# Two blocks of routing arithmetic moved ahead of the first expert tile: the "gate" and "slot row" steps on the Vector engine, and the writes of their results on the Scalar engine's queue

## The chip, the cores and the metric

The kernel runs on one core of one Trainium2 chip. A core has five engines with a queue of instructions each: the tensor engine (PE; its weight loads are listed as PEld), the Vector engine (DVE), the Scalar engine (ACT), GpSimd (POOL) and the Sync engine (SP), which here only starts transfers. Engines run side by side and wait for one another through semaphores. The metric is the device time of one execution in microseconds (us).

## The reference

Three networks in a row, all in 32-bit floating point, on 8 x 576 = 4608 tokens of width 512 (8 heads of 64):

```python
p_packed = sm_attn(p, k, v)              # 32 packed queries per head look at 576 keys
x = sm_attn(q, p_packed, p_packed)       # 576 queries look at the 32 packed rows
# mixture of experts: 8 experts, each token goes to one
logits = x @ w_gate
expert_idx = np.argmax(logits, axis=1)
probs = softmax(logits); gate_w = probs[token, expert_idx]
for e in range(8):
    out[mask_e] = gate_w[mask_e] * (relu(x[mask_e] @ w1[e]) @ w2[e])    # 512 -> 1024 -> 512
# dense layer
h = out @ w_in                           # 512 -> 2048
return (s * relu(h)**2 + b) @ w_out      # 2048 -> 512
```

## The kernel before

There are three stages, and each is written out for every engine as its own program.

**Attention** (up to about 187 us). 16 units of 4 heads. Along with it the expert of each token is picked, and GpSimd scatters the token rows to a table in DRAM that is sorted by expert (`scatter`, L408).

**Experts** (about 214 to 723 us). The sorted table is cut into slots of 128 rows, 40 of them for these inputs, and each slot belongs to one expert. For a slot `s` the work is a ring:

- Scalar starts the load of the 128 rows (`load(s)`, L854), after reading the row number from a table into a register (L853).
- The tensor engine turns them (`slot_in(s)`, L656).
- Scalar copies the turned rows, rounded to the matmul format, to `xT_hi` (`x_hi(s)`, L858), and Vector subtracts that from the exact values to give `xT_lo` (`x_lo(s)`, L1166). Products of both parts are summed, three matmuls for each product (`split_mm`, L647 to L649).
- The tensor engine multiplies by the first weights (`slot_up(s)`: 24 matmuls in two halves), Scalar applies relu to each half (`relu(s)`, L863), the tensor engine turns the result (`slot_turn`, L691), Scalar and Vector split it (`h_hi`, L868, and `h_lo`, L1172), and the tensor engine multiplies by the second weights (`slot_down`).

`slot_up(s)` waits for `x_lo(s)`, as the semaphore `xlo_done` says. The order on the tensor engine is fixed by the program: slot_in(0), slot_up(0), slot_in(1), slot_turn(0), then a loop of slot_up(s), slot_in(s+1), slot_down(s-1), slot_turn(s).

The weights are split into a high and a low part in the same manner, 8 chunks for an expert. The first ten chunks are split by Scalar (`round_high`, L812) together with GpSimd or, for the last three of them, Vector (`round_low`, L1144). All later ones are GpSimd's (`split`, L389 and L391, two instructions a chunk on SBUF). It may start expert 2 only when expert 0's last slot is through (`release`).

**Routing arithmetic** between the two stages, on Vector. Each instruction is wrapped in `step`, which makes the next instruction wait on the semaphore `rt` until this one has ended. Two groups of it are what the change moves:

- the gates, `reduce_sum` (L1153), add of a small constant (L1154), `reciprocal` (L1155), which need the exponentials that Scalar makes at L888;
- the slot rows, four instructions on a table of 96 x 48 x 7 (L1158, L1160, L1161, L1162), which need only the row number of each token.

Scalar writes both results to DRAM with three transfers each (L899, L902). They are read back at the end of the expert stage only. In this kernel the gates stand on Vector behind `x_lo(0)`, and the slot rows behind `h_lo(0)`; Vector also reads the number of slots into a register (L1175) ahead of `x_lo(0)`. On Scalar, both groups of writes stand behind `h_hi(0)`.

**Dense layer** (from about 727 us): gather of the expert results, then 9 groups of 512 tokens.

Of the kernel before, what the change touches and what calls it, by code (L numbers as in the profile page):

```python
# [9 lines left out]
ALU = mybir.AluOpType  # L10
ACT = mybir.ActivationFunctionType
AX = mybir.AxisListType

P = 128
B, H, S, D = 8, 8, 576, 64
NPK = 32
E = 8
SP_ = 96
# [12 lines left out]
EPS = 1e-9  # L31
# [4 lines left out]
C = N // SP_  # L36
# [18 lines left out]
def build(nc, q, k, v, p, w_gate, w1, w2, w_in, w_out, s_in, b_in, out):  # L55
    rows_dram = nc.dram_tensor("x_by_expert", [E * REG, DM], F32).ap()
    ys_dram = nc.dram_tensor("y_by_slot", [SLOTS * P, DM], F32).ap()
    pos_dram = nc.dram_tensor("slot_row_of_token", [N, 1], I32).ap()
    gate_dram = nc.dram_tensor("gate_of_token", [N, 1], F32).ap()

    ctx = ExitStack()
    with ctx:
        def sb(name, shape, dt=F32, scope=ctx):
            return scope.enter_context(nc.sbuf_tensor(name, shape, dt))

        def sem(name):
            return ctx.enter_context(nc.semaphore(name))
# [30 lines left out]
        eoff = sb("expert_region", [SP_, E])  # L98
# [11 lines left out]
        pos_i = sb("row_of_token_sb", [SP_, C], I32)  # L110
# [36 lines left out]
        c = ExitStack()  # L147
# [7 lines left out]
        mxa = sb("mxa", [SP_, C], scope=c)  # L155
        dl = sb("dl", [SP_, C, E], scope=c)
        el = sb("el", [SP_, C, E], scope=c)
        gate = sb("gate", [SP_, C], scope=c)
# [4 lines left out]
        doff = sb("doff", [SP_, E - 1], scope=c)  # L163
        pos_e = sb("pos_e", [SP_, C, E - 1], scope=c)
        pos_s = sb("pos_s", [SP_, C], scope=c)
        slot_row = sb("slot_row_of_token_sb", [SP_, C], I32, scope=c)
# [8 lines left out]
        c = ExitStack()  # L175
# [55 lines left out]
        rt = sem("rt")  # L231
        rexp = sem("rexp")
        zeros_done, zeroed = sem("zeros_done"), sem("zeroed")
        pos_out, gate_out, tok_in = sem("pos_out"), sem("gate_out"), sem("tok_in")
# [531 lines left out]
        def _(act):  # L766
# [80 lines left out]
            def token_rows(t, c):  # L847
                return t.rearrange("(b p c j) o -> c p b (j o)", b=B, c=3, j=J)[c]


            def load(s):

                row = act.value_load(x_at[0:1, bass.ds(s, 1)], min_val=0, max_val=E * REG - P)  # L853
                act.dma_start(xin[:], rows_dram[bass.ds(row, P), :]).then_inc(xin_in, 16)  # L854

            def x_hi(s):
                act.wait_ge(tx_full, s + 1)
                nc.scalar.copy(xT[0][:], ps[:, TXB, :]).then_inc(xhi_done, 1)  # L858
# [6 lines left out]
            def h_hi(s):  # L865
                for n in range(2):
                    act.wait_ge(th_full, 2 * s + n + 1)
                    nc.scalar.copy(hT[0][:, n * 512:(n + 1) * 512], ps[:, THB + n, :]).then_inc(hhi_done, 1)  # L868
# [19 lines left out]
            nc.scalar.activation(el[:], dl[:], ACT.Exp).then_inc(rexp, 1)  # L888
            x_hi(0)
            load(1)  # L890
            act.wait_ge(tail_zero, 16)

            relu(0)
            x_hi(1)
            load(2)
            h_hi(0)
            act.wait_ge(rt, RT_GATE)
            for c in range(3):
                act.dma_start(token_rows(gate_dram, c), gate[c * NPK:(c + 1) * NPK, :].rearrange("p (b j) -> p b j", b=B)).then_inc(gate_out, 16)  # L899
            act.wait_ge(rt, RT_ROW)  # L900
            for c in range(3):
                act.dma_start(token_rows(pos_dram, c), slot_row[c * NPK:(c + 1) * NPK, :].rearrange("p (b j) -> p b j", b=B)).then_inc(pos_out, 16)  # L902
            with act.Fori(1, before3 + 1) as s:
                relu(s)
                x_hi(s + 1)
# [71 lines left out]
        def _(dve):  # L977
# [122 lines left out]
            def step(ins, mark=None):  # L1100

                done[0] += 1
                ins.then_inc(rt, 1)
                dve.wait_ge(rt, done[0])
                if mark is not None:
                    assert mark == done[0], (mark, done[0])
# [33 lines left out]
            def round_low(n):  # L1140
                dve.wait_ge(hi_done, n + 1)
                dve.wait_ge(conv, n)
                at = n // NCH * WBUF
                nc.vector.tensor_tensor(part(at, 1, n % NCH * CH, CH), raw[n % 2][:], part(at, 0, n % NCH * CH, CH), ALU.subtract).then_inc(conv, 1)  # L1144
# [3 lines left out]
            step(nc.vector.tensor_tensor(dl[:], lg[:], over_e, ALU.subtract), RT_DL)  # L1148
            round_low(EARLY)
            round_low(EARLY + 1)  # L1150
            def gates():
                dve.wait_ge(rexp, 1)
                step(nc.vector.reduce_sum(mxa[:], el[:], AX.X))  # L1153
                step(nc.vector.tensor_scalar_add(mxa[:], mxa[:], EPS))  # L1154
                step(nc.vector.reciprocal(gate[:], mxa[:]), RT_GATE)  # L1155

            def slot_rows():
                step(nc.vector.tensor_tensor(pos_e[:], pos_i[:].unsqueeze(2).to_broadcast([SP_, C, E - 1]),  # L1158
                                             eoff[:, 1:].unsqueeze(1).to_broadcast([SP_, C, E - 1]), ALU.is_ge))
                step(nc.vector.tensor_tensor(pos_e[:], pos_e[:], doff[:].unsqueeze(1).to_broadcast([SP_, C, E - 1]), ALU.mult))  # L1160
                step(nc.vector.reduce_sum(pos_s[:], pos_e[:], AX.X))  # L1161
                step(nc.vector.tensor_tensor(slot_row[:], pos_i[:], pos_s[:], ALU.subtract), RT_ROW)  # L1162

            def x_lo(s):
                dve.wait_ge(xhi_done, s + 1)
                nc.vector.tensor_tensor(xT[1][:], ps[:, TXB, :], xT[0][:], ALU.subtract).then_inc(xlo_done, 1)  # L1166

            def h_lo(s):
                for n in range(2):
                    cols = slice(n * 512, (n + 1) * 512)  # L1170
                    dve.wait_ge(hhi_done, 2 * s + n + 1)
                    nc.vector.tensor_tensor(hT[1][:, cols], ps[:, THB + n, :], hT[0][:, cols], ALU.subtract).then_inc(hlo_done, 1)  # L1172

            dve.wait_ge(tables, 1)
            before3 = dve.value_load(slots_m3[0:1, 0:1], min_val=N // P - 3, max_val=SLOTS - 3)  # L1175
            x_lo(0)
            gates()
            x_lo(1)
            h_lo(0)
            slot_rows()  # L1180
            with dve.Fori(1, before3 + 2) as s:
                x_lo(s + 1)
                h_lo(s)
# [50 lines left out]
RT_GATE = 19  # L1234
RT_ROW = 23
# [21 lines left out]
```

## Time and profile before

| | |
|---|---|
| median of 3 runs | 1572.74 us (1571.44 to 1578.85) |
| the profiled execution's own time | 1572.74 us |
| its span, from first to last instruction | 1571.0 us |
| tensor engine busy | 1471.6 us, 94% of the span |
| Vector busy | 483.4 us, 31% |
| Scalar busy | 468.8 us, 30% |
| GpSimd busy | 408.9 us, 26% |

The span is 1.7 us shorter than the execution's time; what is ahead of the first and behind the last instruction is in the time alone. An engine that isn't the tensor engine costs time only where the tensor engine waits for it, so what is to be looked for is where the tensor engine stands idle and what ended that idle time. Line numbers in rows are those of the kernel before. An instruction's own wait is noted behind it in brackets.

### The profile page before, as it was taken

How to read it: one execution, taken by the hardware profiler on the slowest of the kernel's cores; microseconds unless marked ns; L12 is line 12 of the kernel's file. 1: busy time of each engine (PE TensorE's matmuls, PEld its weight loads, DVE VectorE, ACT ScalarE, POOL GpSimd, SP SyncE). 2: the span in 40 equal slices, each digit the busy share in tenths (PEclk: the TensorE clock that was granted, in tenths of full speed). 3: DMA queues.
4: the chain of work that ended last, by engine and by line, in shares of the span. 5: the costliest groups of instructions: out<-in, count | busy, mean ns of one | idle time of the engine just before them, and what ended most of it. 6: DMA issues, size and time to landing. Idle time of an engine off the chain costs nothing.

```text
span 1571.0 us, 24276 instructions
## 1 busy us (share of the span) xinstructions
PE 1471.6 (94%) x8664; PEld 1180.9 (75%) x8665; DVE 483.4 (31%) x777; ACT 468.8 (30%) x793; POOL 408.9 (26%) x268
## 2 busy tenths in 40 slices
PE   7787549999999999995999999999999999999998
PEld 5565438888888888884788888888888888888886
DVE  4767831111111111111523232232323223232322
ACT  6554212222222222221222232232223222222222
POOL 0343559356275666205600000000000000000000
PEclk9878669999999999997999999999999999999999
DMA  9768465233242343212201000010101001000000
GB/s 276 233 218 237 126 223 166 90 121 117 76 147 94 114 132 107 87 35 94 67 7 41 14 35 13 13 40 7 40 13 40 7 13 40 7 33 0 27 0 27
DMA packets 51917, 124.75 MB, mean 79 GB/s; under 512 B 8224, under 2 KB 14368, under 8 KB 50720
## 3 DMA queue, kind: packets, MB, share of 16 engines
q1 hardware_dynamic: 31904, 83.13, 16.6%
q10 hardware_dynamic: 14016, 22.10, 4.4%
q0 software_dynamic: 5952, 18.88, 3.9%
q8 instruction: 33, 0.54, 0.1%
q14 instruction: 12, 0.10, 0.0%
HBM read 90.76 MB, written 33.33 MB: 79 GB/s over the span
## 4 chain that ended last, share of the span: by engine, by line
PE 92%; DVE 3%; issue 2%; DMA 1%; ACT 1%; POOL 1%; ACTq 0%; DVEq 0%; POOLq 0%; SPq 0%
PE psum L647 18%; PE psum L649 18%; PE psum L648 18%; PE psum L727 9%; PE psum L728 9%; PE psum L729 9%; PE psum L486 2%; PE psum L691 2%; PE psum L715 1%; PE psum L656 1%; PE psum L592 1%; PE psum L550 1%; PE psum L529 1%; PE psum L605 1%; DVE x_rows L1067 1%
## 5 line engine op out<-in xcount | busy, mean ns | idle before, releaser
L1195 DVE SCALAR_TENSOR_TENSOR s_r_r<-r_relu,s_col 128x512 f32<-128x512 f32 x144 | 112.8, 784 | 452.2 <-ACT r_relu L937 452.2
L647 PE MATMUL psum<-weights_split,gT_hi 128*128 128x512 f32 x576 | 229.8, 399 | 1.9 <-DVE gT_lo L1197 1.9
L727 PE MATMUL psum<-yT_hi,weights_split 128*128 128x512 f32 x576 | 228.2, 396 | 1.4 <-issue 1.4
L728 PE MATMUL psum<-yT_lo,weights_split 128*128 128x512 f32 x576 | 228.3, 396 | 0.0
L729 PE MATMUL psum<-yT_hi,weights_split 128*128 128x512 f32 x576 | 228.1, 396 | 0.0
L648 PE MATMUL psum<-weights_split,gT_hi 128*128 128x512 f32 x576 | 227.3, 395 | 0.0
L649 PE MATMUL psum<-weights_split,gT_lo 128*128 128x512 f32 x576 | 227.2, 394 | 0.0
L937 ACT ACTIVATE r_relu<-psum 128x512 f32<-128x512 f32 x144 | 86.0, 597 | 464.4 <-PE psum L729 464.4
L389 POOL TENSOR_TENSOR weights_split<-weights_raw,one 128x1024 fp32r<-128x1024 f32 x70 | 134.7, 1924 | 253.2 <-PE psum L649 236.1
L450 POOL DMA_INDIRECT y_gathered<-y_by_slot,tpos x36 | 34.4, 956 | 579.3 <-PE psum L715 577.3
L391 POOL TENSOR_TENSOR weights_split<-weights_raw,weights_split 128x1024 fp32r<-128x1024 f32 x70 | 169.4, 2419 | 5.5
L1197 DVE SCALAR_TENSOR_TENSOR gT_lo<-s_r_r,b_col,gT_hi 128x512 fp32r<-128x512 f32 x144 | 112.7, 783 | 114.1 <-ACT gT_hi L940 114.1
L940 ACT ACTIVATE gT_hi<-s_r_r,b_col 128x512 fp32r<-128x512 f32 x144 | 104.3, 724 | 123.3 <-DVE s_r_r L1195 123.3
L647 PE MATMUL psum<-weights_split,xT_hi 128*128 x320 | 130.6, 408 | 2.9 <-DVE xT_lo L1166 2.9
L647 PE MATMUL psum<-weights_split,hT_hi 128*128 x320 | 129.5, 405 | 2.5 <-DVE hT_lo L1172 2.5
L727 PEld LDWEIGHTS psum<-yT_hi,weights_split 128*128 128x128 f32 x576 | 108.7, 189 | 27.9 <-issue 1.8
L647 PEld LDWEIGHTS psum<-weights_split,gT_hi 128*128 128x128 f32 x576 | 108.3, 188 | 27.4 <-issue 2.1
L729 PEld LDWEIGHTS psum<-yT_hi,weights_split 128*128 128x128 f32 x576 | 108.7, 189 | 26.2
L728 PEld LDWEIGHTS psum<-yT_lo,weights_split 128*128 128x128 f32 x576 | 108.6, 189 | 26.2
L649 PEld LDWEIGHTS psum<-weights_split,gT_lo 128*128 128x128 f32 x576 | 108.1, 188 | 25.7
L649 PE MATMUL psum<-weights_split,xT_lo 128*128 x320 | 127.3, 398 | 0.0
L648 PE MATMUL psum<-weights_split,xT_hi 128*128 x320 | 127.1, 397 | 0.0
(142 smaller groups left out, 1796.8 us busy)
## 6 DMA issues: line engine op xcount, KB each, us to landing
weights_raw<-in_moe_w_dram SPq DMA_DIRECT2D x64, 512.0 KB, 3.4
x_slot<-x_by_expert ACTq DMA_DIRECT2D x40, 256.0 KB, 2.7
y_by_slot<-y_slot ACTq DMA_DIRECT2D x40, 256.0 KB, 2.0
k_sb<-in_k_dram SPq DMA_DIRECT2D x16, 576.0 KB, 6.7
q_sb<-in_q_dram SPq DMA_DIRECT2D x16, 576.0 KB, 7.2
v_sb<-in_v_dram SPq DMA_DIRECT2D x48, 192.0 KB, 5.6
out_dram<-out_sb SPq DMA_DIRECT2D x9, 1024.0 KB, 3.8
weights_raw<-in_moe_w_in_dram SPq DMA_DIRECT2D x8, 512.0 KB, 3.6
```

Source lines behind the costliest of these rows:

```text
L389: nc.gpsimd.tensor_tensor(hi, raw[c_ % 2][:], one[:].to_broadcast([P, CH]), ALU.mult).then_inc(hi_done, 1)
L391: nc.gpsimd.tensor_tensor(lo, raw[c_ % 2][:], hi, ALU.subtract).then_inc(conv, 1)
L647: nc.tensor.matmul(dst, lhs[0][:, col:col + P], rhs[0], start=first_, stop=False)
L648: nc.tensor.matmul(dst, lhs[0][:, col:col + P], rhs[1], start=False, stop=False)
L649: return nc.tensor.matmul(dst, lhs[1][:, col:col + P], rhs[0], start=False, stop=last_)
L727: nc.tensor.matmul(ps[:, HFB + f % 2, :], w[0], yT[0][:, k_, :], start=(k_ == 0), stop=False)
L728: nc.tensor.matmul(ps[:, HFB + f % 2, :], w[0], yT[1][:, k_, :], start=False, stop=False)
L729: last = nc.tensor.matmul(ps[:, HFB + f % 2, :], w[1], yT[0][:, k_, :], start=False, stop=(k_ == KD - 1))
L937: nc.scalar.activation(rel[:], ps[:, HFB + par, :], ACT.Relu).then_inc(rel_done, 1)
L940: nc.scalar.activation(gT[par][0][:], sq[par][:], ACT.Identity, bias=b_col[:]).then_inc(ghi_done, 1)
L1195: nc.vector.scalar_tensor_tensor(sq[par][:], rel[:], s_col[:], rel[:], ALU.mult, ALU.mult).then_inc(sq_done, 1)
L1197: nc.vector.scalar_tensor_tensor(gT[par][1][:], sq[par][:], b_col[:], gT[par][0][:], ALU.add, ALU.subtract).then_inc(glo_done, 1)
```

## The change

On Vector, the gates and the slot rows lose their functions and stand in the program where these were defined: right behind the last `round_low`, ahead of the register load and of `x_lo(0)`. On Scalar, the six writes with their two waits stand behind `load(1)`, ahead of `relu(0)`. No instruction is added or removed.

```diff
             x_hi(0)
             load(1)
-            act.wait_ge(tail_zero, 16)
-
-            relu(0)
-            x_hi(1)
-            load(2)
-            h_hi(0)
             act.wait_ge(rt, RT_GATE)
             for c in range(3):
                 act.dma_start(token_rows(gate_dram, c), gate[...]).then_inc(gate_out, 16)
             act.wait_ge(rt, RT_ROW)
             for c in range(3):
                 act.dma_start(token_rows(pos_dram, c), slot_row[...]).then_inc(pos_out, 16)
+
+            act.wait_ge(tail_zero, 16)
+
+            relu(0)
+            x_hi(1)
+            load(2)
+            h_hi(0)
             with act.Fori(1, before3 + 1) as s:
...
             round_low(EARLY)
             round_low(EARLY + 1)
-            def gates():
-                dve.wait_ge(rexp, 1)
-                step(nc.vector.reduce_sum(mxa[:], el[:], AX.X))
-                step(nc.vector.tensor_scalar_add(mxa[:], mxa[:], EPS))
-                step(nc.vector.reciprocal(gate[:], mxa[:]), RT_GATE)
-
-            def slot_rows():
-                step(... pos_e, is_ge ...)
-                step(... pos_e, mult ...)
-                step(nc.vector.reduce_sum(pos_s[:], pos_e[:], AX.X))
-                step(... slot_row, subtract ..., RT_ROW)
+            dve.wait_ge(rexp, 1)
+            step(nc.vector.reduce_sum(mxa[:], el[:], AX.X))
+            step(nc.vector.tensor_scalar_add(mxa[:], mxa[:], EPS))
+            step(nc.vector.reciprocal(gate[:], mxa[:]), RT_GATE)
+
+            step(... pos_e, is_ge ...)
+            step(... pos_e, mult ...)
+            step(nc.vector.reduce_sum(pos_s[:], pos_e[:], AX.X))
+            step(... slot_row, subtract ..., RT_ROW)
...
             dve.wait_ge(tables, 1)
             before3 = dve.value_load(slots_m3[0:1, 0:1], ...)
             x_lo(0)
-            gates()
             x_lo(1)
             h_lo(0)
-            slot_rows()
             with dve.Fori(1, before3 + 2) as s:
```

On Vector, the program around the start of the expert stage was this. `mxa` and `el` belong to the gates, `pos_e`, `pos_s` and `slot_row_of_token_sb` to the slot rows, and TENSOR_LOAD is the register load.

```order
L1144 TENSOR_TENSOR weights_split<-weights_raw,weights_split 128x1024 [waits conv,hi_done]
L1175 TENSOR_LOAD slots_minus [waits tables]
L1175 ISA x2
L1166 TENSOR_TENSOR xT_lo<-psum,xT_hi 128x512 [waits xhi_done]
L1153 TENSOR_REDUCE mxa<-el 96x48 [waits rexp]
L1154 TENSOR_SCALAR mxa<-mxa 96x48 [waits rt]
L1155 RECIPROCAL gate<-mxa 96x48 [waits rt]
L1166 TENSOR_TENSOR xT_lo<-psum,xT_hi 128x512 [waits xhi_done,rt]
L1172 TENSOR_TENSOR hT_lo<-psum,hT_hi 128x512 [waits hhi_done] x2
L1158 TENSOR_TENSOR pos_e<-row_of_token_sb,expert_region 96x336
L1160 TENSOR_TENSOR pos_e<-pos_e,doff 96x336 [waits rt]
L1161 TENSOR_REDUCE pos_s<-pos_e 96x48 [waits rt]
```

Now it is this (line numbers are the changed kernel's, one or so off from the ones above). All seven instructions have moved ahead of the first `x_lo`, and the register load between them and it has got the wait for `rt`, the end of the last of the seven, besides the one it had.

```order
L1145 TENSOR_TENSOR weights_split<-weights_raw,weights_split 128x1024 [waits conv,hi_done]
L1153 TENSOR_REDUCE mxa<-el 96x48 [waits rexp]
L1154 TENSOR_SCALAR mxa<-mxa 96x48 [waits rt]
L1155 RECIPROCAL gate<-mxa 96x48 [waits rt]
L1157 TENSOR_TENSOR pos_e<-row_of_token_sb,expert_region 96x336 [waits rt]
L1159 TENSOR_TENSOR pos_e<-pos_e,doff 96x336 [waits rt]
L1160 TENSOR_REDUCE pos_s<-pos_e 96x48 [waits rt]
L1161 TENSOR_TENSOR slot_row_of_token_sb<-row_of_token_sb,pos_s 96x48 [waits rt]
L1175 TENSOR_LOAD slots_minus [waits tables,rt]
L1175 ISA x2
L1166 TENSOR_TENSOR xT_lo<-psum,xT_hi 128x512 [waits xhi_done] x2
```

On Scalar, from the exponential on, before:

```order
L888 ACTIVATE el<-dl 96x384 [waits rt]
L858 CAST xT_hi<-psum 128x512 [waits tx_full]
L854 DMA x_slot<-x_by_expert 128x512
L863 ACTIVATE h_relu<-psum 128x512 [waits h_full,tail_zero]
L863 ACTIVATE h_relu<-psum 128x512 [waits h_full]
L868 CAST hT_hi<-psum 128x512 [waits th_full] x2
L899 DMA gate_of_token<-gate 32x8x6 [waits rt]
L902 DMA slot_row_of_token<-slot_row_of_token_sb 32x8x6 [waits rt]
```

And now:

```order
L888 ACTIVATE el<-dl 96x384 [waits rt]
L858 CAST xT_hi<-psum 128x512 [waits tx_full]
L854 DMA x_slot<-x_by_expert 128x512
L893 DMA gate_of_token<-gate 32x8x6 [waits rt]
L893 DMA gate_of_token<-gate 32x8x6 x2
L896 DMA slot_row_of_token<-slot_row_of_token_sb 32x8x6 [waits rt]
L896 DMA slot_row_of_token<-slot_row_of_token_sb 32x8x6 x2
```

Both groups of writes are now ahead of the first relu, with the two waits for Vector.

## Rows read from the trace of the kernel before

**Rows 1.** Stretches: busy us of PE, PEld, DVE, ACT, POOL; granted clock, DMA share, GB/s.

```profile
199.60:213.90 14.30, 0.00 (x0) 0.00 (x0) 1.22 (x1) 1.67 (x2) 0.92 (x1) 0.50 0.97 318
216.60:221.60 5.00, 4.91 (x12) 3.87 (x13) 1.59 (x3) 0.00 (x0) 4.92 (x3) 0.50 0.54 168
227.40:700.00 472.60, 472.60 (x2266) 387.56 (x2267) 80.05 (x118) 124.98 (x225) 253.07 (x119) 1.00 0.34 108
742.30:747.30 5.00, 4.99 (x12) 3.94 (x13) 0.00 (x0) 0.00 (x0) 4.92 (x3) 0.51 0.20 60
```

**Rows 2.** The chain that ended last, 199 to 225 us: start, duration, what.

```profile
199.70 7.99 DMA x_by_expert<-x_rows,row_of_token_sb
...
215.71 0.70 DVE xT_lo L1166
...
216.69 0.79 PE psum L647
217.48 0.43 PE psum L648
...
222.65 0.23 PE psum L647
```

**Rows 3.** Vector in order of time: start, duration, line, operation.

```profile
214.36 1.22 DVE L1144 TENSOR_TENSOR weights_split<-weights_raw,weights_split 128x1024 fp32r<-128x1024 f32 x1 [2.46 <-ACT weights_split L812]
...
216.32 0.54 DVE L1153 TENSOR_REDUCE mxa<-el 96x48 f32<-96x384 f32 x1
216.89 0.88 DVE L1154 TENSOR_SCALAR mxa<-mxa 96x48 f32<-96x48 f32 x1
217.81 0.45 DVE L1155 RECIPROCAL gate<-mxa 96x48 f32<-96x48 f32 x1
...
228.10 1.08 DVE L1158 TENSOR_TENSOR pos_e<-row_of_token_sb,expert_region 96x336 f32<-96x336 int32 x1
229.21 2.08 DVE L1160 TENSOR_TENSOR pos_e<-pos_e,doff 96x336 f32<-96x336 f32 x1
...
231.86 1.75 DVE L1162 TENSOR_TENSOR slot_row_of_token_sb<-row_of_token_sb,pos_s 96x48 int32<-96x48 int32 x1
```

**Rows 4.** Vector's sequencer, line 1175: durations ns min/median/max, start us.

```profile
L1175 DVEq TENSOR_LOAD <-slots_minus x1: 542/542/542, 214.4 to 214.4; - x1
L1175 DVEq FUSED_REGOPS  x1: 221/221/221, 214.9 to 214.9; - x1
L1175 DVEq SEQ_ASSERT  x1: 35/35/35, 215.2 to 215.2; - x1
```

**Rows 5.** GpSimd in order of time, 215 to 243 us.

```profile
215.84 1.89 POOL L389 TENSOR_TENSOR weights_split<-weights_raw,one 128x1024 fp32r<-128x1024 f32 x1 [15.22 <-DVE weights_split L1144]
217.81 2.37 POOL L391 TENSOR_TENSOR weights_split<-weights_raw,weights_split 128x1024 fp32r<-128x1024 f32 x1
...
226.44 2.38 POOL L391 TENSOR_TENSOR weights_split<-weights_raw,weights_split 128x1024 fp32r<-128x1024 f32 x1
228.77 2.16 POOL L389 TENSOR_TENSOR weights_split<-weights_raw,one 128x1024 fp32r<-128x1024 f32 x1
231.01 2.54 POOL L391 TENSOR_TENSOR weights_split<-weights_raw,weights_split 128x1024 fp32r<-128x1024 f32 x1
...
242.16 1.91 POOL L389 TENSOR_TENSOR weights_split<-weights_raw,one 128x1024 fp32r<-128x1024 f32 x1
```

**Rows 6.** Vector and GpSimd in the attention stage, at 69 us.

```profile
69.30 2.37 POOL L382 TENSOR_TENSOR weights_split<-weights_raw,weights_split 128x1024 fp32r<-128x1024 f32 x1
69.40 2.34 DVE L996 TENSOR_TENSOR eq<-logits,mx 96x48 f32<-96x48 f32 x1
```

**Rows 7.** Scalar and its queue (ACTq) in order of time.

```profile
222.06 0.60 ACT L863 ACTIVATE h_relu<-psum 128x512 f32<-128x512 f32 x1 [6.38 <-PE psum L649]
...
233.64 1.36 ACTq L902 DMA_DIRECT2D slot_row_of_token<-slot_row_of_token_sb  x3
235.19 1.09 ACT L863 ACTIVATE h_relu<-psum 128x512 f32<-128x512 f32 x2 [7.84 <-issue]
```

More of the change, by code:

```diff
@@ L1150, in _ @@
             round_low(EARLY + 1)
-            def gates():
-                dve.wait_ge(rexp, 1)
-                step(nc.vector.reduce_sum(mxa[:], el[:], AX.X))
-                step(nc.vector.tensor_scalar_add(mxa[:], mxa[:], EPS))
-                step(nc.vector.reciprocal(gate[:], mxa[:]), RT_GATE)
-            def slot_rows():
-                step(nc.vector.tensor_tensor(pos_e[:], pos_i[:].unsqueeze(2).to_broadcast([SP_, C, E - 1]),
-                                             eoff[:, 1:].unsqueeze(1).to_broadcast([SP_, C, E - 1]), ALU.is_ge))
-                step(nc.vector.tensor_tensor(pos_e[:], pos_e[:], doff[:].unsqueeze(1).to_broadcast([SP_, C, E - 1]), ALU.mult))
-                step(nc.vector.reduce_sum(pos_s[:], pos_e[:], AX.X))
-                step(nc.vector.tensor_tensor(slot_row[:], pos_i[:], pos_s[:], ALU.subtract), RT_ROW)
+            dve.wait_ge(rexp, 1)
+            step(nc.vector.reduce_sum(mxa[:], el[:], AX.X))
+            step(nc.vector.tensor_scalar_add(mxa[:], mxa[:], EPS))
+            step(nc.vector.reciprocal(gate[:], mxa[:]), RT_GATE)
+            step(nc.vector.tensor_tensor(pos_e[:], pos_i[:].unsqueeze(2).to_broadcast([SP_, C, E - 1]),
+                                         eoff[:, 1:].unsqueeze(1).to_broadcast([SP_, C, E - 1]), ALU.is_ge))
+            step(nc.vector.tensor_tensor(pos_e[:], pos_e[:], doff[:].unsqueeze(1).to_broadcast([SP_, C, E - 1]), ALU.mult))
+            step(nc.vector.reduce_sum(pos_s[:], pos_e[:], AX.X))
+            step(nc.vector.tensor_tensor(slot_row[:], pos_i[:], pos_s[:], ALU.subtract), RT_ROW)
             def x_lo(s):
```

## The prediction

> **What bounds the kernel now.** I read the busy shares first (tensor engine 94%), then the stretches, then the chain, then each engine in order of time around the two places that the change touches. From 227.4 to 700 us the tensor engine is busy for all of 472.6 us, at full granted clock [rows 1]. In that stretch no other engine costs anything, and none can give anything back by being early. The hole is ahead of it: from 199.6 to 213.9 us the tensor engine does nothing, and the granted clock is 0.50, the lower of its two levels [rows 1]. The chain says what ends the hole [rows 2]: GpSimd's last scatter at 199.70 and its transfer of 7.99 us, then the first slot's load, turn and copy, then Vector's x_lo(0) at 215.71 for 0.70, then 0.27 of issue, and at 216.69 the first matmul of slot_up(0). So x_lo(0) is on the path that sets the end. In the kernel before, Vector had nothing in front of it but the last round_low, which starts at 214.36 and takes 1.22 [rows 3]. The seven moved instructions come behind x_lo(0) there, in time in which Vector only waited for others. The change puts them in front of it.
>
> **Where the block starts.** The last round_low ends at 214.36 + 1.22 = 215.58. I start the block at 215.52, as an in-order successor of this instruction overlaps it by some hundredths. The exponentials that it waits for come from Scalar ahead of x_hi(0), so they are there by then.
>
> **How long it takes.** Here the recorded durations can't be copied, as some of them are waiting. L1154 works on 48 elements a partition and is recorded with 0.88; it ends at 216.89 + 0.88 = 217.77 [rows 3]. GpSimd's L389 runs from 215.84 to 217.73 [rows 5]: Vector's instruction ends 0.04 behind it. L1158 ends at 229.18, 0.36 behind the end of GpSimd's L391 (226.44 + 2.38 = 228.82). L1160 ends at 231.29, 0.36 behind L389's (228.77 + 2.16 = 230.93), and L1162 at 233.61, 0.06 behind L391's (231.01 + 2.54 = 233.55). The same is seen in the attention stage, where a comparison of 48 elements lasts 2.34 and ends at 71.74, behind a GpSimd instruction that ends at 71.67 [rows 6]. I read from this that these four of the seven wait until the GpSimd instruction that is under way has ended, and that between two of them GpSimd gets in the next of its own. The two reductions and the reciprocal don't wait (0.54 for L1153 and 0.45 for L1155 [rows 3]).
>
> The Trainium skill has this rule, under "SBUF — State Buffer", section "SBUF: two separate sides": GpSimd and those Vector instructions that have two SBUF inputs or run in a 2-port mode share one pair of ports by an exclusive lock, and whoever comes second waits for the whole instruction of the other. The trace agrees, with the 2.34 above. By this rule the moved block is to be timed against GpSimd's instructions, as I do next; by the recorded lengths alone it would come out 2 us shorter, the first of the rivals below.
>
> So I step through it. GpSimd's first split starts at 215.84, released by the last round_low, and that doesn't move.
> - L1153: 215.52 to 216.06.
> - L1154: from 216.09, waits for GpSimd's L389, ends at 217.77 as before. L1155: 217.81 to 218.26 [rows 3].
> - L1158: from 218.30, waits for L391 (217.81 + 2.37 = 220.18 [rows 5]), and ends 0.36 later, at 220.54.
> - L1160: its end was 231.29 - 229.18 = 2.11 behind that of L1158, with one L389 between, and the same order holds here: 222.65.
> - L1161 and L1162 together: 233.61 - 231.29 = 2.32, with one L391 between: 224.97.
>
> **The register load.** Before, Vector's sequencer read the slot count (L1175) at 214.4, for 542 + 221 + 35 ns, while round_low was running [rows 4]: 0.84 from its start to its end, handovers included, and wholly hidden. In the changed program it waits for the last of the seven. Nothing covers it there, so 224.97 + 0.02 + 0.84 = 225.83, and x_lo(0) starts at about 225.87. Bounds for what of it shows: 0 and 0.9. I take the 0.84, as the semaphore wait stands on that instruction.
>
> **The sum.** x_lo(0) moves from 215.71 to 225.87, that is by 10.16 us. The block takes 224.97 - 215.52 = 9.45, of which its four waits for GpSimd are 1.64 + 1.88 + 1.72 + 1.68 = 6.9 and its own work and gaps 2.5; the register load with its handovers adds 0.90; and 0.19 goes off, as the block starts that much ahead of where x_lo(0) stood. The first matmul moves with it from 216.69 to 226.85, as nothing else is later: x_hi(0) is done on time, the weights of expert 0 have been split, and this hole is only getting longer.
>
> **Terms costed at nothing.**
> - Clock. slot_up(0) begins at the lower level: its matmuls are 0.43 apart at 217.5 and 0.23 at 222.65 [rows 2], and 12 are in that first stretch [rows 1]. At 742 us, after another pause, it is 12 again in 5 us at 0.51 [rows 1]. The clock was already at 0.50 in the hole, so a longer hole doesn't lower it. Bounds: none of the 24 slow, -12 x 0.20 = -2.4, or all, +2.4. I take 0, as both recoveries agree.
> - Scalar. It now waits for the end of the slot rows, 224.97, and issues three writes (1.36 [rows 7]): free at about 226.5. Queued behind is relu(0), at 222.06 before; its input comes 10.16 later, at 232.2. So 5.7 us of cover; without it, each us past it would be a us more. The gates' writes go at 218.3, and load(1) is ahead of them all. No transfer passes another on Sync's or GpSimd's queue. The six small writes now share the engines with other weight chunks; before, GpSimd did not wait for a chunk in this stretch, so 0, and at most some tenths through the lock.
> - Scalar's wait of 7.84 ahead of relu(1), at 235.19 [rows 7], goes away. It gives nothing: the tensor engine was busy throughout [rows 1].
> - GpSimd. Its next expert may start when slot 0 is through. It started at 242.16 right behind the split before it [rows 5], so slot 0 was through by then. Slot 0's end moves by 10.16, to 252.3 at the latest: GpSimd will wait there, and it starts later by 10.2 at most, no more than the slots that need those weights.
> - The rest of the run, behind 227.4, is shifted as a whole.
>
> The profiled execution's own time is 1572.74 us, its span and 1.7 around it, and it is also the median of the runs. 1572.74 + 10.16 = 1582.9.
>
> **The rivals.**
> 1. The block costs what its rows say: 1.94 for the gates and 5.51 for the slot rows, x_lo(0) at 223.0, and with the register load 223.9: +8.2, 1580.9; if the load hides after all, +7.3, 1580.1. For it: these are the rows. Against it: the ends that fall on GpSimd's. Chance 0.11.
> 2. The other side, not slower: Vector gets its port before GpSimd does, since it is already running when GpSimd's first split starts at 215.84, and GpSimd queues behind it. All four waits are then gone, 10.16 - 6.9 = +3.3, 1576.0. This would decide from about two waits saved on: with more than 2.3 us of the 6.9 gone the change is within what can't be told from nothing. For it: the first start is only 0.25 from L1154's. Against it: L1160 and L1162 came to a GpSimd that had got in between. Chance 0.05.
> 3. Scalar's relief is worth something: relu(1) could have run at about 227.4 + 12 x 0.23 = 230.2 in place of 235.19. If a later load or relu hung on it, 5.0 would come back: +5.2, 1577.9. Against it: no idle time on the tensor engine from 227.4 on. Chance 0.04.
> 4. One turn more: one of the four misses its gap and waits for another GpSimd instruction, 2.4: +12.6, 1585.3. Chance 0.08.
>
> **How the numbers follow.** My forecast has 0.72 and runs from 1582 to 1584.5 by itself, with the spread of a median. The range should leave out no more than 2 in 10: it takes in rival 1's upper half and rival 4, so 1579.8 to 1586.2. What a measurement of this kernel can tell from no change is 0.5%, 7.9 us, or 1580.6. Slower by more: 0.72 x 0.93 + 0.11 x 0.5 + 0.08 = 0.80. Within: 0.18, from the rest of these, and rivals 2 and 3. Faster has no mechanism, 0.02 for a measurement that strays.
>
> **What would show it.** In the profile of the changed kernel: x_lo(0) at about 225.9 and the first matmul of slot_up(0) at 226.9; the four instructions ending just behind GpSimd's; the register load between the last of them and x_lo(0); Scalar's first relu still waiting for the tensor engine; a new wait of GpSimd at 242; the stretch behind busy throughout; 12 slow matmuls. The forecast is wrong if x_lo(0) is at 223 or 219, or if the tensor engine has a new idle time in the slots behind slot 1.

## The result and the profile after

| | before | changed |
|---|---|---|
| median (20 runs each) | 1575.11 us (1570.46 to 1581.74) | 1583.68 us (1577.95 to 1591.67) |
| ratio | | 1.0053, 95% interval 1.0042 to 1.0065 |
| profiled execution's own time, span | 1572.74, 1571.0 us | 1581.47, 1579.7 us |

The changed kernel is 8.4 us slower (6.6 to 10.2). Against the 1572.74 that the forecast starts from, its median is +10.9, inside the range; against the median of all 20 runs of before it is +8.6.

In the profiles the start of the expert stage itself moves from execution to execution, by the length of all that lies ahead. So positions are compared against the start of the last `round_low` ahead of x_lo(0) (L1144 of before, L1145 here), where the two programs part. In before it is at 214.36, here at 213.15, so this execution came 1.2 us earlier to that point. Vector in order of time (start, duration, line, operation; in brackets idle time and what ended it):

```profile
213.15 1.23 DVE L1145 TENSOR_TENSOR weights_split<-weights_raw,weights_split 128x1024 fp32r<-128x1024 f32 x1 [2.77 <-ACT weights_split L812]
214.29 0.55 DVE L1153 TENSOR_REDUCE mxa<-el 96x48 f32<-96x384 f32 x1
214.87 1.70 DVE L1154 TENSOR_SCALAR mxa<-mxa 96x48 f32<-96x48 f32 x1
216.60 0.45 DVE L1155 RECIPROCAL gate<-mxa 96x48 f32<-96x48 f32 x1
217.09 2.22 DVE L1157 TENSOR_TENSOR pos_e<-row_of_token_sb,expert_region 96x336 f32<-96x336 int32 x1
219.34 2.08 DVE L1159 TENSOR_TENSOR pos_e<-pos_e,doff 96x336 f32<-96x336 f32 x1
221.45 0.50 DVE L1160 TENSOR_REDUCE pos_s<-pos_e 96x48 f32<-96x336 f32 x1
221.99 1.70 DVE L1161 TENSOR_TENSOR slot_row_of_token_sb<-row_of_token_sb,pos_s 96x48 int32<-96x48 int32 x1
224.64 0.69 DVE L1166 TENSOR_TENSOR xT_lo<-psum,xT_hi 128x512 fp32r<-128x512 f32 x1 [0.96 <-DVE slot_row_of_token_sb L1161]
```

And GpSimd over the same stretch:

```profile
214.63 1.89 POOL L389 TENSOR_TENSOR weights_split<-weights_raw,one 128x1024 fp32r<-128x1024 f32 x1 [15.73 <-DVE weights_split L1145]
216.60 2.34 POOL L391 TENSOR_TENSOR weights_split<-weights_raw,weights_split 128x1024 fp32r<-128x1024 f32 x1
218.90 2.16 POOL L389 TENSOR_TENSOR weights_split<-weights_raw,one 128x1024 fp32r<-128x1024 f32 x1
221.13 2.48 POOL L391 TENSOR_TENSOR weights_split<-weights_raw,weights_split 128x1024 fp32r<-128x1024 f32 x1
...
248.22 1.89 POOL L389 TENSOR_TENSOR weights_split<-weights_raw,one 128x1024 fp32r<-128x1024 f32 x1 [7.38 <-PE psum L649]
```

Read the two side by side. L1154 ends at 216.57, behind GpSimd's 216.52; L1157 at 219.31, 0.37 behind 218.94; L1159 at 221.42, 0.36 behind 221.06; L1161 at 223.69, 0.08 behind 223.61. L1154, which was recorded with 0.88 in [rows 3], now has 1.70 for the same 48 elements, since it starts 0.24 behind the start of GpSimd's instruction, where in [rows 3, 5] it was 1.05.

Vector's sequencer, line 1175 (durations in ns, then start):

```profile
L1175 DVEq TENSOR_LOAD <-slots_minus x1: 547/547/547, 223.7 to 223.7; - x1
L1175 DVEq FUSED_REGOPS  x1: 221/221/221, 224.3 to 224.3; - x1
L1175 DVEq SEQ_ASSERT  x1: 35/35/35, 224.6 to 224.6; - x1
```

The same three steps as in [rows 4], now in the 0.96 that Vector idles between the last of the seven and x_lo(0). x_lo(0) starts 224.64 - 213.15 = 11.49 behind round_low, against 215.71 - 214.36 = 1.35 in [rows 2, 3]: 10.14 later. The stretches that answer to [rows 1] (columns as there), and the tensor engine's first matmul:

```profile
216.60:225.50 8.90, 0.00 (x0) 0.00 (x0) 7.63 (x6) 0.00 (x0) 8.79 (x4) 0.50 0.44 125
225.58:230.30 4.72, 4.72 (x11) 3.76 (x12) 0.00 (x0) 0.00 (x0) 4.64 (x3) 0.50 0.54 155
236.20:710.00 473.80, 473.80 (x2271) 388.52 (x2272) 74.78 (x114) 125.22 (x225) 243.03 (x115) 1.00 0.31 106
```

```profile
225.58 0.79 PE L647 MATMUL psum<-weights_split,xT_hi 128*128 x1 [11.74 <-DVE xT_lo L1166]
```

The hole has grown at its end by a stretch in which only Vector and GpSimd work. 11 matmuls are at the lower clock level (0.50), and from 236.2 to 710 us the tensor engine is busy throughout: nothing is given back there. Scalar (its queue is ACTq) shows that its own part is free:

```profile
223.72 1.37 ACTq L896 DMA_DIRECT2D slot_row_of_token<-slot_row_of_token_sb  x3
230.87 0.60 ACT L863 ACTIVATE h_relu<-psum 128x512 f32<-128x512 f32 x1 [16.39 <-PE psum L649]
```

The last write is issued at 225.1, and the relu behind it waits for the tensor engine until 230.87.

### The profile page after: what moved, and what is told of

Read it like the earlier page. It is cut to its first block, busy times and chain, and to the rows that moved or that the text cites. A ratio compares the mean times of both kernels' runs of the same rounds, so it can differ in the third digit from the quotient of the medians.

```text
span 1579.7 us, 24276 instructions
## 1 busy us (share of the span) xinstructions
PE 1471.8 (93%) x8664; PEld 1181.3 (75%) x8665; DVE 486.1 (31%) x777; ACT 469.3 (30%) x793; POOL 408.8 (26%) x268
## 4 chain that ended last, share of the span: by engine, by line
PE 91%; DVE 4%; issue 2%; DMA 1%; ACT 1%; SPq 0%; POOL 0%; DVEq 0%; ACTq 0%; POOLq 0%
PE psum L647 18%; PE psum L649 18%; PE psum L648 18%; PE psum L727 9%; PE psum L728 8%; PE psum L729 8%; PE psum L486 2%; PE psum L691 2%; PE psum L715 1%; PE psum L656 1%; PE psum L592 1%; PE psum L550 1%; PE psum L529 1%; DMA weights_raw<-in_moe_w_dram 1%; DVE x_rows L1068 1%
## 5 line engine op out<-in xcount | busy, mean ns | idle before, releaser
L389 POOL TENSOR_TENSOR weights_split<-weights_raw,one 128x1024 fp32r<-128x1024 f32 x70 | 134.7, 1924 | 263.9 <-PE psum L649 247.5
```

The source lines that it names most:

```text
L389: nc.gpsimd.tensor_tensor(hi, raw[c_ % 2][:], one[:].to_broadcast([P, CH]), ALU.mult).then_inc(hi_done, 1)
```

## The experiments

The measure in the first column of numbers is the start of x_lo(0) minus the start of the last round_low, in us. The second is the ratio to runs of the kernel before on the same chip; 0.001 is 1.6 us.

| kernel | x_lo(0) behind round_low | ratio (95%) |
|---|---|---|
| before; before_again | 1.35; 1.35 | 1.0004 (0.9991 to 1.0016) |
| changed; after_again; after_third | 11.49; 11.50; 11.49 | 1.0053; 1.0051 (1.0029 to 1.0073); 1.0068 (1.0046 to 1.0089) |
| gates_early | 4.86 | 1.0015 (0.9997 to 1.0034) |
| rows_early | 6.97 | 1.0037 (1.0018 to 1.0057) |
| gpsimd_held | 5.18 | 1.0012 (0.9992 to 1.0033) |
| scalar_as_before | 11.49 | 1.0068 (1.0044 to 1.0092) |
| read_ahead | 10.57 | 1.0025 (1.0012 to 1.0038) |
| idle_block | 1.35 | 0.9985 (0.9966 to 1.0004) |
| tail_late | 1.6 | 0.9959 (0.9941 to 0.9978) |
| idle_tail | 1.7 | 0.9976 (0.9958 to 0.9993) |

### gpsimd_held: are the four slow, or do they wait?

```diff
             pool.wait_ge(conv, EARLY + 2)
+            pool.wait_ge(rt, RT_ROW)
             for n in range(EARLY + 2, 2 * NCH):
```

> The changed kernel, but GpSimd starts its first weight split only when the slot rows are done. Theory 1 (four of the seven wait for GpSimd's port): these four drop to 0.2 (48 elements) and 0.4 to 0.5 (336 elements), the block from 9.4 to 2.9, x_lo(0) at 1.15 + 2.9 + 0.9 = 4.9 behind the last round_low's start in place of 11.49, time +3.6 against the kernel before. GpSimd's splits start 1.6 later than in the changed kernel, with cover. Rival (the instructions are slow by themselves, for their broadcast or integer operands): block 9.4 as in the changed kernel, time +10.1 or more, as GpSimd's weights are then late by 10.

```profile
219.27 0.18 DVE L1155 TENSOR_SCALAR mxa<-mxa 96x48 f32<-96x48 f32 x1
219.49 0.45 DVE L1156 RECIPROCAL gate<-mxa 96x48 f32<-96x48 f32 x1
219.97 0.50 DVE L1158 TENSOR_TENSOR pos_e<-row_of_token_sb,expert_region 96x336 f32<-96x336 int32 x1
220.51 0.50 DVE L1160 TENSOR_TENSOR pos_e<-pos_e,doff 96x336 f32<-96x336 f32 x1
...
221.57 0.20 DVE L1162 TENSOR_TENSOR slot_row_of_token_sb<-row_of_token_sb,pos_s 96x48 int32<-96x48 int32 x1
```

With GpSimd quiet the four take 0.18, 0.50, 0.50 and 0.20 in place of 1.70, 2.22, 2.08 and 1.70. The reciprocal and the reductions are as before. So they wait, and the waiting is 11.49 - 5.18 = 6.3 us of the loss. The 4.9 of the expectation became 5.18, as the block took 221.77 - 218.69 = 3.08 in place of 2.9 and the register load 0.95. The instructions show the same without being moved or held: in tail_late (below), where they stand as in the kernel before and GpSimd happens to be idle up to 233.71, L1158 took 0.49 at 232.95 and L1160 0.51 at 233.48, for 1.08 and 2.08 in [rows 3]. By the Trainium skill, "SBUF — State Buffer", section "SBUF: two separate sides", the loser of the shared port pair blocks for the whole of the other's instruction; this trace and the changed kernel's agree, with those pairs of numbers.

### gates_early and rows_early: the block in parts

In gates_early only `gates()` stands ahead of the register load, in rows_early only `slot_rows()` (with the two marks of `rt` swapped); Scalar's program is the kernel before's in both.

```diff
+            gates()            # rows_early: slot_rows()
             dve.wait_ge(tables, 1)
             before3 = dve.value_load(...)
             x_lo(0)
-            gates()
```

> Only the gates (3 instructions) stand ahead of x_lo(0); slot rows and Scalar's program are the kernel before's. The measure is the start of x_lo(0) minus the start of the last round_low: 1.35 us in the kernel before, 11.49 in the changed one. Theory 1 (one of the three waits for the GpSimd instruction under way, and the register load of 0.84 shows behind the last of them): gates of 3.4 us in the changed trace (214.29 to 217.05 and its handover), then the load, so 1.2 + 2.8 + 0.9 = 4.9, time +3.5. Rival (what costs is the slot rows or Scalar's wait for them, gates are free as their input is early): about 1.4, time +0. Rival 2 (the register load stays hidden): 4.0, time +2.7.

> Only the slot rows (4 instructions) stand ahead of x_lo(0); gates behind it and Scalar's program as in the kernel before. Same measure. Theory 1: the first of them (1.14 behind the start of the last round_low) starts some 0.3 before GpSimd's first split and so runs without a wait for 0.4, the second waits for the end of GpSimd's first instruction (3.4 behind round_low's start) and ends at 3.9, the reduction at 4.4, the fourth waits for the next GpSimd instruction and ends at about 6.2, and with the load x_lo(0) is at 7.0: time +5.7. Rival (each instruction takes what its row before says, 5.51 in all): 1.15 + 5.51 + 0.9 = 7.6, time +6.2; and the first one would be as long as before, 1.08.

In rows_early, Vector:

```profile
212.00 0.50 DVE L1158 TENSOR_TENSOR pos_e<-row_of_token_sb,expert_region 96x336 f32<-96x336 int32 x1
212.53 2.08 DVE L1160 TENSOR_TENSOR pos_e<-pos_e,doff 96x336 f32<-96x336 f32 x1
```

and GpSimd:

```profile
212.34 1.91 POOL L389 TENSOR_TENSOR weights_split<-weights_raw,one 128x1024 fp32r<-128x1024 f32 x1 [14.99 <-DVE weights_split L1144]
```

4.86 and 6.97 were measured for 4.9 and 7.0. Their ratios, 1.0015 and 1.0037, are 2.4 and 5.8 us, where +3.5 and +5.7 were expected. The first slot-row instruction, which starts 0.34 ahead of GpSimd's, doesn't wait; the next, 0.19 behind it, does, and ends 0.36 behind GpSimd's end at 214.25. The recorded length of such an instruction says when it came in relation to the other engine, not what it costs.

### scalar_as_before: does Scalar's part cost anything?

Vector's program is the changed one; on Scalar the writes stand behind `h_hi(0)`, as in the kernel before.

> Vector's program is the changed one, Scalar's program is the kernel before's (writes behind h_hi(0)). Theory 1 (all of the loss is Vector's block and the register load behind it): x_lo(0) 11.5 behind the last round_low's start, time as the changed kernel's, +10.1 by the trace and +8.4 by the ratio of many runs. Rival (Scalar's waits and writes ahead of the first relu cost part of it): faster than the changed kernel by 1 us or more, and the first relu earlier against slot_up(0)'s first half.

11.49, and no faster than the changed kernel (1.0068, with an interval from 1.0044, for 1.0053). The first relu comes 5.4 behind the start of slot_up(0) for 5.3 in the changed kernel. Scalar's part costs nothing that shows.

### read_ahead: the register load

```diff
             round_low(EARLY + 1)
+            dve.wait_ge(tables, 1)
+            before3 = dve.value_load(slots_m3[0:1, 0:1], ...)
             dve.wait_ge(rexp, 1)
             (the seven)
-            dve.wait_ge(tables, 1)
-            before3 = dve.value_load(slots_m3[0:1, 0:1], ...)
             x_lo(0)
```

> The changed kernel with the register load ahead of the seven instructions in place of behind them. Theory 1 (the load of 0.84 is exposed in the changed kernel only because it waits for the last of the seven): it runs under round_low as in the kernel before, x_lo(0) is 10.55 behind the last round_low's start in place of 11.49, time 0.9 below the changed kernel's. Rival (the 0.95 between the last of the seven and x_lo(0) is Scalar's x_hi or a semaphore): 11.49 as before.

```profile
224.99 1.70 DVE L1163 TENSOR_TENSOR slot_row_of_token_sb<-row_of_token_sb,pos_s 96x48 int32<-96x48 int32 x1
226.72 0.69 DVE L1168 TENSOR_TENSOR xT_lo<-psum,xT_hi 128x512 fp32r<-128x512 f32 x1
```

x_lo(0) follows within 0.03, the idle 0.96 is gone, and the measure is 10.57. The ratio fell further than 0.9 us accounts for (its interval ends at 1.0038, where 9.2 us would be 1.0058); the trace has no place for more, and why stays open.

### idle_block: the same seven, in Vector's idle time ahead of the round_low of chunk 8

```diff
             step(... dl ..., RT_DL)
+            slot_rows()
+            gates()
             round_low(EARLY)
             round_low(EARLY + 1)
```

with the exponential ahead of Scalar's wait for the scatters, the writes where the kernel before has them, and the two marks of `rt` swapped.

> The seven instructions stand in Vector's idle time of 11 us ahead of the round_low of chunk 8, the exponential on Scalar ahead of its wait for the scatters, the writes where the kernel before has them. Theory 1: GpSimd does no arithmetic there, so the seven take about 2.9 as in gpsimd_held, and all of it is hidden; x_lo(0) is 1.35 behind the last round_low's start, the time is the kernel before's. Scalar doesn't stall ahead of relu(1), which gives nothing. Rival (Vector's work there slows GpSimd's last scatters or the chain in front of the first slot): round_low later against the last scatter by up to 3, time +1 to +3.

```profile
201.02 0.50 DVE L1156 TENSOR_TENSOR pos_e<-row_of_token_sb,expert_region 96x336 f32<-96x336 int32 x1
201.55 0.50 DVE L1158 TENSOR_TENSOR pos_e<-pos_e,doff 96x336 f32<-96x336 f32 x1
...
211.53 1.23 DVE L1144 TENSOR_TENSOR weights_split<-weights_raw,weights_split 128x1024 fp32r<-128x1024 f32 x1 [7.00 <-ACT weights_split L812]
```

All seven run at their bare length in time that Vector idles, 7.0 us of which are left. The measure is 1.35 and no difference in time can be told. From the last scatter to round_low it is 216.66 - 201.12 = 15.5, where before has 14.7 and other kernels with an unchanged program up to there have 14.4 to 15.6. Moving this work early costs nothing that shows if it is early enough (the interval ends at 1.0004); the change put it in the last place before x_lo(0).

### tail_late and idle_tail: what sets the hole itself

```diff
-            sp.dma_start(ys_dram[N:SLOTS * P, :]..., zeros...).then_inc(tail_zero, 16)
             for n in range(EARLY + 1, 2 * NCH):
                 chunk(n % NCH, n, expert_chunk(n // NCH, n % NCH))
+                if n == EARLY + 3:
+                    sp.dma_start(ys_dram[N:SLOTS * P, :]..., zeros...).then_inc(tail_zero, 16)
```

and Scalar's `wait_ge(tail_zero, 16)` in front of its loop of slots. idle_tail is this with idle_block.

> The kernel before, but Sync's transfer of zeros into the last slots of the result table (1.8 MB) is started behind the load of weight chunk 11 in place of ahead of chunk 8, and Scalar waits for it ahead of the loop of slots in place of ahead of relu(0). The DMA engines are busy 0.97 to 0.99 in the hole ahead of slot 0, so if bandwidth sets its length, 1.8 MB at the 300 GB/s of that stretch is up to 6 us: from the last scatter to the last round_low 9 to 12 in place of 14.7, time -3 to -6. Rival (the latency of the scatter and of the row load sets it, not bandwidth): 14.7 as before, time +0.

> idle_block and tail_late together. Theory 1: the seven instructions stay hidden and the late zeros save what they saved alone, 0.41%, so 0.994 to 0.997 of the kernel before; slot_up(0) some 13.4 behind the last scatter in place of 17.0, and a wait of about 2 for weights at slot_up(1), since the next chunks come late. Rival (the seven need the bandwidth or the ports that the shorter hole has less of): slower than tail_late by 1 us or more.

The zeros were a part of what fills the DMA engines in the hole: their busy share from the last scatter to the first slot's transposes is 0.97 in before (199.70 to 213.94) and 0.72 in tail_late (208.95 to 219.59). In tail_late the first matmul of slot_up(0) comes 222.31 - 208.95 = 13.4 behind the start of the last scatter, in before 216.69 - 199.70 = 17.0 (17.3 in before_again); in idle_tail it is 210.63 - 196.35 = 14.3, for 17.8 in idle_block. Tensor engine in tail_late:

```profile
222.31 0.79 PE L648 MATMUL psum<-weights_split,xT_hi 128*128 x1 [1.60 <-DVE xT_lo L1166]
...
232.74 0.50 PE L648 MATMUL psum<-weights_split,xT_hi 128*128 x1 [1.80 <-POOL weights_split L392]
```

Vector in tail_late, the two rounds_low in one row:

```profile
218.47 2.55 DVE L1144 TENSOR_TENSOR weights_split<-weights_raw,weights_split 128x1024 fp32r<-128x1024 f32 x2 [9.67 <-ACT weights_split L813]
221.36 0.69 DVE L1166 TENSOR_TENSOR xT_lo<-psum,xT_hi 128x512 fp32r<-128x512 f32 x1 [0.33 <-ACT xT_hi L859]
```

The last round_low takes 1.23, so it starts at 218.47 + 2.55 - 1.23 = 219.8, 10.8 behind the last scatter (9 to 12 expected, 14.7 in before). x_lo(0) comes 1.6 behind it, as it now waits 0.33 for x_hi(0). At slot_up(1) the tensor engine waits 1.80 for GpSimd's weights, which are loaded later; in before it waits 1.27 there for x_lo(1), so some 0.5 comes back. In idle_tail that wait is 1.36, and not the 2 that was expected.

Both kernels beat the kernel before: tail_late by 0.41%, which is 6.5 us (3.5 to 9.3), idle_tail by 0.24%, 3.8 us (1.1 to 6.6). For tail_late -3 to -6 was expected. The traces account for 3.1 to 3.4 in tail_late and for 2.7 to 3.5 in idle_tail. The ratio of tail_late rests on 7 executions, and what it has beyond the trace isn't explained. idle_tail was expected at 0.994 to 0.997 and came out at 0.9976. Whether it is slower than tail_late, as its rival said, can't be told, as the intervals overlap.

### before_again, after_again, after_third: 8.4 measured, 10.1 in the traces

> The changed kernel once more, for its time. By the traces so far, the start of the last round_low lies between 210.9 and 218.0 us from execution to execution, whatever the kernel, and all behind it repeats within 0.3 us; against it x_lo(0) is 10.1 later. Theory 1 (nothing comes back, the 8.4 of the first measurement is 10.1 with the scatter of the attention stage): a mean ratio between 1.0053 and 1.0070, nearer to 1.0064 with more runs, and 11.5 from round_low to x_lo(0). Rival (1.7 us comes back somewhere): 1.0053 again, and in the trace a stretch ahead of round_low or behind slot_up(0) that is shorter.

> The kernel before, against itself. The changed kernel was 1.0053 and 1.0051 of it, 8.2 us, where the traces say 10.1. Theory A (in some executions the first slot's rows arrive later than the last round_low ends, which costs the kernel before and is hidden in the changed one): x_lo(0) more than 1.35 behind the last round_low's start in this trace, by 1 to 3. Theory B (it is the scatter of the attention stage's length): 1.35 again, a ratio within 0.2% of 1, and a start of the last round_low anywhere from 210 to 219.

> The changed kernel a third time. Theory B: 11.5 from the last round_low to x_lo(0), and the mean of the three ratios between 1.005 and 1.0068. Theory A: the same in the trace, ratio 1.005.

before_again shows the 1.35 once more:

```profile
212.95 1.23 DVE L1144 TENSOR_TENSOR weights_split<-weights_raw,weights_split 128x1024 fp32r<-128x1024 f32 x1 [3.02 <-ACT weights_split L812]
214.30 0.69 DVE L1166 TENSOR_TENSOR xT_lo<-psum,xT_hi 128x512 fp32r<-128x512 f32 x1
```

Theory A isn't seen: in both traces of before x_hi(0) is done within 0.1 us of round_low's end. Theory B holds as far as the runs go. Weighted by their intervals, the three ratios of the changed kernel make 1.0055, which is 8.7 us, give or take 1.5, and 10.1 lies in that, near its upper end. The expectation of after_again, a mean ratio of 1.0053 to 1.0070, was just missed (1.0052 for the first two). The traces show nothing that comes back: from the first matmul of slot_up(0) to the end it is 1354.3 and 1358.0 us in the two of before, and 1354.1, 1356.0 and 1357.5 in the three of the changed kernel. As these scatter by 4 us, that 1 us of the 10.1 comes back isn't excluded.

## Why the prediction was right, step by step

- **The bound** (x_lo(0) ends the hole, all behind it is full): right. PE's idle 11.74 is put down to x_lo, and 236.2 to 710 is busy throughout.
- **Start and length of the block**: 9.45 forecast, 223.69 - 214.29 = 9.40 measured. All four turns fell where the stepping put them, and gpsimd_held shows that the waits are what they were taken for. The four waits were put at 6.9; with GpSimd quiet 6.3 go, as some 0.14 in each of what I took for waiting is the instruction's own work (0.18 for 0.04, 0.50 for 0.36).
- **The register load**: 0.90 with handovers forecast, 0.95 measured from 223.69 to 224.64, 0.92 taken away by read_ahead.
- **The sum**: x_lo(0) +10.16 forecast, +10.14 measured against round_low. The mechanism and its size are right, by the traces.
- **Costed at nothing**: Scalar's part (scalar_as_before), its old stall of 7.84 (idle_block took it away and gained nothing that shows), GpSimd's new wait (7.38, up to 248.22, which against round_low is 7.3 later than the same instruction in [rows 5]; at most 10.2 was forecast). GpSimd pays for the shared port too: its L389 at 218.90 has 2.16 for 1.89, within the forecast's some tenths. The clock: 11 of slot_up(0)'s matmuls are followed at the lower level's distance of some 0.4 us in both kernels (the 12 of the forecast counts one that the next follows after 0.26), and from slot_up(0) to slot_up(1) it is 10.60 for 10.68. Over all traces here there are 7 to 13 such matmuls and 10.05 to 11.11 us, so the two equal recoveries that the forecast leaned on were in part luck: this term is worth half a us either way from one execution to the next.
- **The rivals**: rival 1 (recorded lengths) would have had x_lo(0) at 9.5 behind round_low (223.9 against 214.36); 11.49 rules it out. The time alone would not have: its +8.2 lies nearer to the measured 8.4 than the forecast's 10.16. (Its lower figure is 1580.0 and not 1580.1, and both figures lie in the range, not the upper half only.) Rival 2 (Vector ahead of GpSimd) did not happen in the changed kernel, and rows_early shows half of its mechanism: one instruction, 0.34 early, went free, though GpSimd's has 1.91 for 1.89 and hardly waited. In tail_late both halves show: GpSimd's instruction at 233.71, which came 0.23 behind the start of L1160, has 2.03 for 1.89, and L1160 went free. The moved block has the reduction first, and that used up this lead. Rivals 3 and 4 weren't seen.
- **Where the forecast was off**: its base. 1572.74 was a low draw of a kernel whose median over 20 runs is 1575.11. Of the 10.9 between that base and the new median, 2.4 is this, and the measured effect is 8.4 for 10.16. Its interval just reaches 10.1; the traces carry the size, the ratio its sign. That the new median lies inside the forecast's own 1582 to 1584.5 is in part luck: the low base and the small measured effect offset each other.

## What to carry to other kernels

An instruction's recorded length on Vector may be mostly a wait for GpSimd: before moving it, step it through GpSimd's instructions at its new place, and take its work from an occurrence with GpSimd quiet. Small work that is hidden behind the first item of a pipeline becomes latency when it is put in front of it, and a register load behind it is exposed along with it; look for idle time ahead of both. When executions scatter by more than the effect, measure positions against a common point of the two traces.

## What I had not expected of the hardware

- The start of the last round_low lay between 210.9 and 218.4 us in the traces of kernels whose programs are the same up to there, and slot_up(0) to the first dense matmul took 524.9 to 527.9: the second of these was expected to repeat within 0.3 us and doesn't. What makes this 3 us was not looked for.
- The first slot's transposes started 0.63 to 0.68 behind the start of Scalar's copy of chunk 9 in all traces in which the zeros are sent early, though the two wait for different transfers on different queues (213.94 and 213.28 in before, 217.97 and 217.34 in after_again). With the zeros late this is no longer so: in tail_late the transposes start at 219.59 and the copy of chunk 9 at 218.3, which is 1.3.
